# Softmax of the first three groups in halves of four heads, and accumulators copied out bank by bank ahead of the attention work

## The reference

```
# q, k, v: 4 x 8 heads x 576 x 64
scores = q @ k.T / 8, only for 0 <= query - key < 64, else -1e9
attn = exp(scores - rowmax);  attn = attn / (rowsum + 1e-9);  x = attn @ v   # -> 2304 x 512
h = x @ w_in_a;   g = s * relu(h)**2 + b;                  x2  = g @ w_out_a  # 512 -> 2048 -> 512
h = x2 @ w_in_b;  g = max(h, 0) + alpha * min(h, 0);       out = g @ w_out_b
```

## Time and profile before

| | |
|---|---|
| median of 3 runs | 909.94 us (909.58 to 910.25) |
| the profiled execution | 910.64 us, its span 908.9 us |
| TensorE busy | 886.0 us, 97% of the span |
| VectorE, ScalarE, POOL busy | 410.2, 285.9, 91.5 us |
| granted TensorE clock | 1.00 |
| first `down` | 55.3 us after the span's start |

### The profile page before, as it was taken

How to read it: one execution, slowest core, us unless ns; L and a number is a source line. 1 busy time by engine, 2 the same in 40 slices (tenths; PEclk the granted TensorE clock), 3 DMA queues, 4 the chain that set the end, 5 groups by cost and what they waited for, 6 DMA issues and landing times.

```text
span 908.9 us, 13847 instructions
## 1 busy us (share of the span) xinstructions
PE 886.0 (97%) x5664; PEld 831.9 (92%) x5664; DVE 410.2 (45%) x945; ACT 285.9 (31%) x717; POOL 91.5 (10%) x81
## 2 busy tenths in 40 slices
PE   4799999999999999999999999999999999999998
PEld 4799999999999999999999999999999999999987
DVE  5155544444444444444354444454453444444443
ACT  4156543434434443444455211111121111111111
POOL 5135500000000000000356200000000000000000
PEclk9999999999999999999999999999999999999999
DMA  6425421102112110300344200200200200200000
GB/s 232 167 79 166 123 87 54 53 25 78 39 53 88 53 53 24 129 6 1 122 124 127 93 0 1 70 1 1 70 1 1 70 0 1 70 1 1 35 1 35
DMA packets 18767, 53.06 MB, mean 58 GB/s; under 512 B 2064, under 2 KB 2064, under 8 KB 18704
## 3 DMA queue, kind: packets, MB, share of 16 engines
q1 hardware_dynamic: 18704, 52.18, 17.5%
HBM read 42.74 MB, written 9.44 MB: 57 GB/s over the span
## 4 chain that ended last, share of the span: by engine, by line
PE 91%; ACT 4%; DVE 3%; DMA 1%; issue 1%; DVEq 0%
PE hid L252 44%; PE acc L297 22%; PE acc L291 20%; PE bank_x L334 2%; ACT p L392 2%; PE bank_x L313 1%; DMA qk<-in_qk 1%; PE bank_x L322 1%; PE bank_y L322 1%; DVE relu L474 1%; ACT g L377 1%; DVE g L488 1%; DVE p L518 1%; ACT relu L367 1%; PE acc L322 0%
## 5 line engine op out<-in xcount | busy, mean ns | idle before, releaser
L252 PE MATMUL hid<-x,w_in 128*128 128x384 f32 (+1 forms) x2352 | 447.8, 340 | 4.5 <-DVE x L530 4.5
L252 PEld LDWEIGHTS hid<-x,w_in 128*128 128x128 f32 x2352 | 418.1, 193 | 16.1 <-DVE x L530 5.1
L291 PE MATMUL acc<-g,w_out 128*128 128x384 f32 x1152 | 223.6, 337 | 2.7 <-ACT outs L426 2.7
L297 PE MATMUL acc<-w_out,g 128*128 128x512 f32 x864 | 215.4, 393 | 0.4 <-DVE g L492 0.4
L291 PEld LDWEIGHTS acc<-g,w_out 128*128 128x128 f32 x1152 | 199.8, 188 | 4.8 <-issue 3.8
L297 PEld LDWEIGHTS acc<-w_out,g 128*128 128x128 f32 x864 | 160.7, 188 | 30.0 <-DVE g L492 0.8
L380 ACT ACTIVATE g<-relu 128x384 fp32r<-128x384 f32 x96 | 50.4, 525 | 332.7 <-DVE relu L482 332.7
L474 DVE SCALAR_TENSOR_TENSOR relu<-relu,consts 128x384 f32<-128x384 f32 x96 | 71.0, 739 | 165.6 <-ACT relu L367 165.6
L479 DVE TENSOR_SCALAR relu<-hid,consts 128x384 f32<-128x384 f32 x96 | 59.3, 617 | 161.5 <-PE hid L252 161.5
L488 DVE SCALAR_TENSOR_TENSOR g<-relu,consts,g 128x384 fp32r<-128x384 f32 x96 | 59.9, 624 | 65.8 <-ACT g L377 65.8
L367 ACT ACTIVATE relu<-hid 128x384 f32<-128x384 f32 x96 | 46.8, 488 | 132.6 <-PE hid L252 132.6
(11 more groups left out here) (54 smaller groups left out, 314.6 us busy)
## 6 DMA issues: line engine op xcount, KB each, us to landing
qk<-in_qk SPq DMA_DIRECT2D x18, 640.0 KB, 5.0
v<-in_v SPq DMA_DIRECT2D x18, 512.0 KB, 3.6
x_scratch<-outs SPq DMA_DIRECT2D x6, 768.0 KB, 4.0
qk<-x_scratch SPq DMA_DIRECT2D x6, 768.0 KB, 5.7
piece<-in_w_in_a SPq DMA_DIRECT2D x16, 256.0 KB, 2.8
piece<-in_w_out_a SPq DMA_DIRECT2D x16, 256.0 KB, 3.0
piece<-in_w_in_b SPq DMA_DIRECT2D x16, 256.0 KB, 2.8
piece<-in_w_out_b SPq DMA_DIRECT2D x16, 256.0 KB, 2.6
```

The costliest lines, as they stand in the source:

```text
L252: mm = pe.matmul(hid[f % 2][:, at], w_in[:, wi, f, dc, :], x[:, par, xi, dc, at], start=(dc == 0 and n == 0), stop=(dc == ND - 1 and n == 2))
L291: mm = pe.matmul(acc[dc][:, 0:TILE], w_out[:, wi, f, dc * 128:(dc + 1) * 128], g[:, f % 2, gi, :], start=(f == 0 and n == 0), stop=(f == N ...
L297: mm = pe.matmul(acc[a][:, :], g[:, f % 2, gi, a * 128:(a + 1) * 128], w_out[:, wi, f, :], start=(f == 0 and n == 0), stop=(f == NF - 1 an ...
```

## The change

**Halves.** For groups 0 to 2 a "part" is half a group, four heads (two of the pairs `u`), so there are six. Each has two banks (`early_banks`): parts 0 and 4 bank_x and bank_y, 1 and 5 acc[0..1], 2 acc[2..3], 3 hid[0..1], with parts 4 and 5 in the upper 256 columns. Every step of a group is there once for a part, with 256 columns instead of 512, or four heads instead of eight, and with semaphores of its own (`e_...`). Maxima of parts 4 and 5 wait for the transposes of parts 0 and 1, since p has two buffers still. Part 4's scores wait for the maxima of part 0, part 5's for those of part 1.

**Loads.** Queries and keys of groups 0 to 2 come in halves; those of group 2 go to `outs`, which is free at the start, and wait for nothing. v of groups 0 and 1 follow, then the pieces; v of group 2, 3 and 4 and queries and keys of 3 and 4 stand ahead of pieces 6 and on.

**Normalising.** POOL multiplies parts 1, 2 and 3 before it turns to its weight pieces, VectorE parts 0, 4 and 5.

**First passes.** `first_ups` is gone; `up(0)`, `scores(3)`, `up(1)`, `up(2)` follow all six parts, in full width.

**Copying out.** `copy_out` stands right behind `lo` and `hi`, ahead of all attention work of the pass. ScalarE has banks 0 and 2, VectorE 1 and 3 (block b: 1), each copy raises its semaphore, and `down` waits before each bank for that bank alone (`acc_free`).

The core of the diff:

```diff
+    POOL_HALVES = (1, 2, 3)
+    DVE_HALVES = (0, 4, 5)
...
+        def early_banks(part):
+            return ((bank_x, bank_y), (acc[0], acc[1]), (acc[2], acc[3]), (hid[0], hid[1]))[part % 4]
+        def early_bank(part, h):
+            at = 256 * (part // 4)
+            return early_banks(part)[h][:, at:at + 256].rearrange("p (u t) -> p u t", u=2)
+        def early_qk(j):
+            return qkv[:, j] if j < 2 else outs[:, 0:PAIRS * QK].rearrange("p (u c) -> p u c", u=PAIRS)
...
-            load_qk(0)
-            load_qk(1)
-            load_v(0)
+            for j in range(NO):
+                early_load_qk(j)
+            early_load_v(0)
+            early_load_v(1)
             load_piece(0)
             load_piece(1)
-            load_v(1)
             sp.dma_start(consts[:, :], consts_in).then_inc(consts_here, 16)
-            load_qk(2)
             load_piece(2)
             load_piece(3)
+            early_load_v(2)
+            load_qk(3)
             load_piece(4)
             load_piece(5)
...
             load_v(3)
             load_qk(4)
             load_v(4)
+            for n in range(6, BY_POOL + SLOTS):
+                load_piece(n)
...
+            for part in POOL_HALVES:
+                j, half = divmod(part, 2)
+                pool.wait_ge(e_rec, part + 1)
+                pool.tensor_tensor(half_heads(j, half), half_heads(j, half), half_rec(j, half),
+                                   ALU.mult).then_inc(e_p_pool, 1)
...
-            for j in range(NO):
-                scores(j)
-            for j in range(NO):
-                transposed(j)
-                values(j)
-                first_ups(j)
-            scores(NO)
+            for part in range(PARTS):
+                early_scores(part)
+            pe.wait_ge(tables, 2)
+            early_transposed(0)
+            for part in range(1, PARTS):
+                early_transposed(part)
+                early_values(part - 1)
+            early_values(PARTS - 1)
+            up(0)
+            scores(NO)
+            up(1)
             up(LAG)
...
+            def acc_free(t, n):
+                if n % 2 == 0:
+                    pe.wait_ge(acc_read_act, 2 * (t - 1) + n // 2 + 1)
+                elif t <= NT:
+                    pe.wait_ge(acc_read_dve, 2 * (t - 1) + n // 2 + 1)
+                else:
+                    pe.wait_ge(acc_read_dve, 2 * NT + t - NT)
...
+                for n in (0, 2):
+                    if t == 2 * NT - 1:
+                        act.wait_ge(last_summed, n + 1)
+                    else:
+                        act.wait_ge(down_done, (t + 1) * NF)
+                    act.activation(outs[:, n * width:(n + 1) * width], acc[n][:, 0:width],
+                                   ACT.Copy).then_inc(last_copied[n] if t == 2 * NT - 1 else acc_read_act, 1)
...
+                if i == NF - 1 and t >= 0:
+                    copy_out(t)
                 if s - 3 in group_at:
                     copy_pt(group_at[s - 3])
...
-                if i == NF - 1 and t >= 0:
-                    copy_out(t)
...
+            early_maxima(0, 0)
+            early_maxima(0, 1)
+            early_sums(0, 0)
+            early_normalise(0, 0)
+            early_maxima(1, 0)
+            early_sums(0, 1)
+            early_maxima(1, 1)
+            early_copy_pt(0, 0)
+            early_sums(1, 0)
+            early_copy_pt(0, 1)
+            early_x_low(0, 0)
+            early_maxima(2, 0)
+            early_sums(1, 1)
+            early_copy_pt(1, 0)
+            early_x_low(0, 1)
+            early_maxima(2, 1)
+            early_sums(2, 0)
+            early_normalise(2, 0)
+            early_x_low(1, 0)
+            early_copy_pt(1, 1)
+            early_x_low(1, 1)
+            early_sums(2, 1)
+            early_normalise(2, 1)
...
```

More of the change, by code:

```diff
@@ new lines, in value, with early_scores @@
+            def value(bank, col, v_of, u):
+                for a in range(2):
+                    for h in range(2):
+                        at = col + WIN * a
+                        mm = pe.matmul(bank[64 * h:64 * h + 64, at:at + WIN],
+                                       v_of[:, a, (2 * u + h) * HD:(2 * u + h + 1) * HD],
+                                       pt[:, h, u, WIN * a:WIN * a + WIN], start=True, stop=True)
+                return mm
+            def early_scores(part):
+                j, half = divmod(part, 2)
+                pe.wait_ge(e_qk_here[j][half], 16)
+                if part >= 4:
+                    pe.wait_ge(e_max, 4 * (part - 3))
+                for n in range(2):
+                    mm = score(early_banks(part), 256 * (part // 4) + 128 * n, early_qk(j), 2 * half + n)
+                mm.then_inc(e_s, 1)
@@ new lines, in early_transposed @@
+            def early_transposed(part):
+                j, half = divmod(part, 2)
+                if part in POOL_HALVES:
+                    pe.wait_ge(e_p_pool, POOL_HALVES.index(part) + 1)
+                else:
+                    pe.wait_ge(e_p_dve, DVE_HALVES.index(part) + 1)
+                for n in range(2):
+                    for h in range(2):
+                        mm = pe.transpose(early_bank(part, h)[:, n, :], p[:, j % 2, 4 * half + 2 * n + h, :], ident[:, :])
+                mm.then_inc(e_pt, 1)
@@ new lines, in early_maxima @@
+            def early_maxima(j, half):
+                if half == 0:
+                    if j:
+                        dve.wait_ge(e_max, HEADS * j)
+                    masked(j)
+                    dve.wait_ge(mask_done, j + 3)
+                dve.wait_ge(e_s, 2 * j + half + 1)
+                if j >= 2:
+                    dve.wait_ge(e_pt, 2 * (j - 2) + half + 1)
+                dve.memset(gate[:, 2 * j + half:2 * j + half + 1], 0.0)
+                for i in range(4 * half, 4 * half + 4):
+                    maximum(j, i, early_bank(2 * j + half, i % 2)[:, i // 2 % 2, :], e_max)
@@ new lines, in early_sums, with early_normalise @@
+            def early_sums(j, half):
+                part, four = 2 * j + half, slice(4 * half, 4 * half + 4)
+                dve.wait_ge(e_exp, 4 * part + 4)
+                dve.tensor_scalar(rowsum[:, j % 2, four], rowsum[:, j % 2, four], 1e-9, None,
+                                  ALU.add).then_inc(e_sum, 1)
+                dve.wait_ge(e_sum, part + 1)
+                dve.reciprocal(rowrec[:, j % 2, four], rowsum[:, j % 2, four]).then_inc(e_rec, 1)
+            def early_normalise(j, half):
+                dve.wait_ge(e_rec, 2 * j + half + 1)
+                dve.tensor_tensor(half_heads(j, half), half_heads(j, half), half_rec(j, half),
+                                  ALU.mult).then_inc(e_p_dve, 1)
```

336 lines of the change are left out of this document (195 added, 141 removed).

## The result

The changed kernel takes 894.14 us (median of 4 runs, 893.55 to 894.55), beside 909.76 for the kernel before in the same series: a ratio of 0.9828, 95% interval 0.9811 to 0.9845. That is 15.6 us less, and 894.8 was forecast. The profiled execution's span went from 908.9 to 892.0 us, 16.9 less. So the sum came out, but the traces show that its terms did not: what I gave to the time before the first `down` was too small by 4.2 us, and 2.6 us that I had priced at nothing were lost again.

A forecast was written before the change was run, and what follows sets the result against it. TensorE was taken to bound the kernel, busy 886.0 of 908.9 us. Gains of 11.7 (start), 3.3 (copies at boundaries) and 0.1 (last copy) sum to 15.1 us, taking the median from 909.94 to 894.8, range 890.8 to 899.2.

The forecast's parts named there:

- TensorE's narrow products: Before the first `down`: 72 narrow `up` products take 16.1 us; `up(0)` and `up(1)` in full width would cost 8.1 or 4.2.
- The layout of the halves: Start, softmax of groups 0 to 2 in six halves: x complete at 31.5 against 43.94 before, bounds 29.5 to 35.
- Port waits: Start, VectorE's sums and normalising of halves 4 and 5 among POOL's weight pieces: 1.3 us, four steps at 0.75 would be 3.0.
- From x to `down`: From x complete to `down(0)`: 12.1 us, bounds 10.1 to 14.0; `down(0)` at 43.6 instead of 55.33, 11.7 us gained.
- rival (a): Start: fast clock during `up(0)` or as it ends, 9.3 to 10.1 us instead of 12.1, time about 892.3; chance 0.20.
- Weights and the first tile, at nothing: First tile: weight pieces arrive in time, the last by about 37, g(0) and g(1) made under `up(1)` and `up(2)`; cost nothing.
- Copies: Tile boundaries: copies ahead of the exponents gain 0.8 us at each of four, 3.3; the very last copy 0.1.
- the cover for g(17): First tile boundary: g(17) ready at 133.8, `down(17)` wants it at 134.9, so 1.0 us of cover is left.
- Sum: Whole kernel: 11.7 + 3.3 + 0.1 = 15.1 us gained, median 894.8 from 909.94.
- (b): Start: softmax by halves slower, POOL's halves at double price and full port waits, x at 35, time 898.3; chance 0.15.
- (c): Tile boundaries: copies bring nothing, `down` waits for g(17) or the new group's transposes instead, time 898.1; chance 0.05.
- (d): Start: POOL's product with a broadcast factor far dearer than the subtraction, slower than before, 914 at 8 us a half; chance 0.05.

## Why the prediction was right, and where its steps were not

- **TensorE's narrow products.** Right: taking them away alone gave 8.7 us. The layout of the halves gave x at 31.5, measured 29.99. Within it POOL's half took 1.04 where I had 1.27, and the first transposes ran at 0.11 each instead of 0.22, as TensorE was at the fast level from about 9.3 to 16.5, which I had not reckoned with.
- **Port waits.** I put 1.3 us on VectorE's sums and normalising of halves 4 and 5. Against the 0.17 and 0.69 of the same steps alone the sums took 0.80 and 0.58 and the normalising 0.82 and 1.62: 2.1 us. The chain's L655 shows the largest. The mechanism was right: the normalising of 22.77 to 24.39 ends 0.55 behind the end of POOL's subtraction (22.58 + 1.26), and the two steps in the first tile 0.4 behind theirs. The Trainium skill ("SBUF — State Buffer", section "Who interferes with whom") has the two take their shared port in turn, an exclusive lock. The trace agrees better with that than with a fixed share: a step begun beside a subtraction ends a little less than its own length behind it, 0.55 of 0.69, 0.4 of 0.62 and 1.1 of 1.22 us. What I did not see, though the layout held it, is that most of the wait of 3.3 us was VectorE's own order: with that changed it is gone, and `up(0)` starts 2.9 us earlier.
- **From x to `down`.** The mis-sized term: 12.1 forecast, 39.27 - 29.99 = 9.3 measured. Here rival (a) came true, with its lower bound of 9.3, though its time of 892.3 did not, as the first tile gave 2.6 us back. The rise came at the end of `up(0)`, and scores(3) and `up(1)` were fast. The row on which the choice rested, 4.04 us of wide products before the rise, would have allowed it; I took the break by scores(3) for a hindrance.
- **Weights and the first tile, at nothing.** Wrong: 2.6 us were given back. The pieces were in time for TensorE, which is all I had asked. I had written down that they end near 37, and that g(0) is made under `up(1)`, but did not lay the two over each other on the port. 1.1 of it went with two loads moved.
- **Copies.** Right: 3.3 + 0.1 forecast, 3.6 measured alone, and the cover for g(17) held.
- **Sum.** 15.1 forecast, 15.6 measured, as the errors on both sides of `down(0)`, +4.2 (15.9 against 11.7) and -2.6, nearly met, with 0.2 to 0.3 more at the boundaries; 1.3 us of the span's 16.9 do not show in the medians. That the forecast lies within 0.7 us of the time is in part luck.
- **Rivals (b), (c), (d).** None came. POOL's product with a broadcast factor was cheaper than the subtraction, not dearer.

## What to carry to other kernels

Matmuls that were put early to fill a pipeline's start have a price on the engine that everything else there goes through; ask what stands behind them, and do them once in full width if the answer is the critical work. When a chain is split into halves on in-order engines, the order on each engine decides more than the length of its steps: lay the steps out in time, and look for a step that is ready long before its turn. And once a start becomes shorter, lay what used to be long done (here POOL's weight pieces) over the elementwise work again, port by port, not only against the engine that uses the result.

## What the runs showed of the hardware

- The same instructions started about 2 us apart in different executions (`up(0)` at 26.27 and 28.07, and at 25.60 and 27.92), with TensorE's clock back at 20 us in one and at 31 in another. Four runs of one variant lie within 0.9 to 3.4 us; the kernel before ran in 907.4 to 910.9.
- Busy time alone did not tell when the clock rises. Narrow products of 128 columns and transposes kept TensorE busy 7.1 of 8 us at a granted clock of 0.5, and it did not rise until `up(2)`. Transposes and values kept it busy 3.75 of 4 us in two other kernels, and it rose in one of them.
- The granted clock in a profile's rows can stay at 1.00 where the durations are those of the slow level (12 products of 384 columns in 4.04 and in 2.08 us, both at 1.00, in the kernel before), so it is worth reading both.
- VectorE and POOL held each other up: a normalising of 1024 columns took 1.97 us instead of 1.22 beside POOL's subtraction, and the subtraction that was begun beside that normalising 2.26 instead of 1.27.
- POOL multiplied 512 columns by a broadcast factor in 1.04 us, and subtracted 512 columns with a rounded result in 1.27.
